# An attention and two MLP blocks on one core: when the first queries, the third weight unit and the last stores are issued

## The reference

```python
# block 1: attention. q, k, v: (4, 8, 1152, 64)
q_pool = q.reshape(B, H, S // 2, 2, D).mean(axis=3)         # 576 pooled queries
scores = matmul(q_pool, k.transpose(0, 1, 3, 2)) / sqrt(D)
attn = exp(scores - max(scores)); attn /= sum(attn) + 1e-9
x = matmul(attn, v)                                         # -> (4, 576, 512)

# block 2: gated MLP that mixes tokens
h = gelu(x @ w_in)                                          # 512 -> 1024
u, v = h[..., :512], h[..., 512:]
v_n = (v - mean) / sqrt(var + 1e-6) * g_ln
v_s = einsum('ts,bsd->btd', w_sg, v_n) + b_sg
x = x + (u * v_s) @ w_out

# block 3: token mixing, then channel mixing
u = x + (relu(x^T @ w_tok1) @ w_tok2)^T                     # 576 -> 256 -> 576
out = u + relu(u @ w_ch1) @ w_ch2                           # 512 -> 1536 -> 512
```

## Time and profile before

| | |
|---|---|
| three runs | 991.78, 992.71, 993.19 us |
| the profiled execution, its own time | 991.15 us |
| its span in the trace | 989.3 us |
| PE busy | 976.6 us, 99% of the span |
| DVE, ACT, POOL busy | 565.7, 462.1, 378.8 us |
| granted TensorE clock | 0.999 of full |
| DMA engines, mean share | 85% in the first fortieth, 30 to 50% through attention, near 0 after |

### The profile page before, as it was taken

The page is one execution under the profiler, slowest core; times in us unless marked ns, Lnnn a source line. Parts: engine busy times, 40 slices in busy tenths (PEclk is TensorE's granted clock), DMA queues, the critical chain, the costliest instruction groups (busy, mean ns, idle before and its releaser), DMA issues.

```text
span 989.3 us, 22718 instructions
## 1 busy us (share of the span) xinstructions
PE 976.6 (99%) x8810; PEld 806.3 (81%) x8810; DVE 565.7 (57%) x1166; ACT 462.1 (47%) x878; POOL 378.8 (38%) x295
## 2 busy tenths in 40 slices
PE   7999999999999999999999999999999999999998
PEld 6777777777777776689999999888888888888898
DVE  5787888888888877787575847545113122131121
ACT  5788888888888877844332423312111111011110
POOL 5777777777777786440000004484000000000000
PEclk9999999999999999999999999999999999999999
DMA  8544444444444433310000002141001001010010
GB/s 251 145 121 120 119 119 119 116 117 111 116 118 117 119 83 97 116 40 1 1 1 1 1 1 57 37 146 43 1 1 43 1 0 42 0 40 3 0 44 22
DMA packets 34459, 65.00 MB, mean 66 GB/s; under 512 B 6256, under 2 KB 15344, under 8 KB 34416
## 3 DMA queue, kind: packets, MB, share of 16 engines
q1 hardware_dynamic: 33968, 63.82, 22.9%
q10 hardware_dynamic: 448, 0.56, 0.2%
HBM read 42.93 MB, written 4.72 MB: 48 GB/s over the span
## 4 chain that ended last, share of the span: by engine, by line
PE 93%; DVE 3%; issue 1%; DMA 1%; POOL 1%; ACT 1%; SPq 0%; ACTq 0%; DVEq 0%; POOLq 0%
PE ps L894 18%; PE ps L895 18%; PE ps L896 18%; PE ps L835 15%; PE ps L823 11%; PE ps L740 8%; PE ps L811 1%; DVE prob L1406 1%; PE ps L813 1%; PE ps L812 1%; DMA k_plain<-in_k 1%; PE ps L950 1%; PE ps L788 1%; POOL prob L627 1%; PE ps L900 0%
## 5 line engine op out<-in xcount | busy, mean ns | idle before, releaser
L627 POOL TENSOR_SCALAR prob<-prob,rsum 128x1152 f32<-128x1152 f32 x144 | 177.7, 1234 | 94.1 <-DVE rsum L1415 94.0
L1406 DVE TENSOR_SCALAR_CACHE_REDUCE prob<-ps 128x1152 f32<-128x1152 f32 x128 | 173.8, 1358 | 65.8 <-PE ps L823 57.6
L1180 ACT ACTIVATE prob<-prob,nmax 128x1152 f32<-128x1152 f32 x144 | 181.3, 1259 | 9.7 <-DVE nmax L1389 4.4
L835 PE MATMUL ps<-pT,v_sb 128*64 128x288 f32 x1152 | 170.6, 418 | 0.0
L1653 DVE SCALAR_TENSOR_TENSOR f_l<-ps,f_h 128x512 fp32r<-128x512 f32 (+1 forms) x60 | 38.3, 638 | 222.4 <-ACT f_h L1350 222.4
L1350 ACT ACTIVATE f_h<-ps 128x512 fp32r<-128x512 f32 (+1 forms) x60 | 33.3, 555 | 254.7 <-PE ps L896 254.7
L1173 ACT ACTIVATE pT<-ps 128x512 f32<-128x512 f32 (+1 forms) x288 | 111.9, 436 | 64.6 <-PE ps L740 56.0
L823 PE MATMUL ps<-k_over,q_over 64*128 64x288 f32 x720 | 127.1, 309 | 0.0
L823 PEld LDWEIGHTS ps<-k_over,q_over 64*128 64x128 f32 x720 | 98.7, 184 | 26.3 <-DVE prob L1406 25.8
L740 PE MATMUL ps<-ident,prob 64*128 64x64 f32 x2592 | 105.2, 222 | 4.1 <-POOL prob L627 2.7
L740 PEld LDWEIGHTS ps<-ident,prob 64*128 64x128 f32 x2592 | 100.7, 139 | 8.9 <-issue 8.9
(11 more groups left out here) (158 smaller groups left out, 2150.6 us busy)
## 6 DMA issues: line engine op xcount, KB each, us to landing
q_raw<-in_q SPq DMA_DIRECT2D x15, 640.0 KB, 5.0
v_sb<-in_v SPq DMA_DIRECT2D x32, 288.0 KB, 2.9
k_raw<-in_k SPq DMA_DIRECT2D x15, 576.0 KB, 4.0
k_over<-kh SPq DMA_DIRECT2D x30, 144.0 KB, 2.5
k_over<-kl SPq DMA_DIRECT2D x30, 144.0 KB, 2.6
out_x<-xT SPq DMA_DIRECT2D x4, 1024.0 KB, 4.2
q_over<-qh SPq DMA_DIRECT2D x30, 128.0 KB, 2.3
q_over<-ql SPq DMA_DIRECT2D x30, 128.0 KB, 2.4
```

Source lines behind the costliest of these rows:

```text
L627: g.tensor_scalar(sl, sl, rsum[:, s:s + 1], 0.0, ALU.mult, ALU.add).then_inc(norm_done, 1)
L835: ins = te.matmul(ps[PH * c:PH * c + PH, ACC_BANK, 0:n], v_sb[:, a, j, :], pT[:, a, j, c * n:c * n + n], start=(j == 0), stop=(j == KB - 1))
L1180: sc.activation(sl, sl, ACT.Exp, scale=-1.0, bias=nmax[:, s:s + 1], accum_out=esum[:, s:s + 1]).then_inc(exp_done, 1)
L1406: ve.tensor_scalar(prob[:, PROB_BUF[s], :].rearrange("p (c n) -> p c n", c=SCORE_BANKS), ps[:, b0:b0 + SCORE_BANKS, 0:CK], -SCALE, BIG, AL ...
```

## The change

1. The queries of tiles 0 and 1 of the first pair are loaded apart: tile 0's ahead of the keys, tile 1's behind them, with a semaphore of their own (`q_next_in`). DVE adds tile 0's halves, POOL tile 1's, and PE's step 1 waits for `q_next_summed`.
2. Head B's keys for `k_plain` are issued ahead of head B's queries. POOL's sum of head B's queries moves from before the first `norm` to behind it. `q_two_b` gets a place of its own beside the rest, since it is now read later.
3. Weight unit 2 is loaded one pair earlier, and units 0 and 1 are split in steps 6 and 7 instead of 7 and 8.
4. Of the last four stores ACT issues the second and the fourth.

```diff
         def load_a(eng, rows, k_to):
-            eng.dma_start(q_two[rows, :, 0:2 * P], q[0, 0:PH, :, 0:2 * P]).then_inc(q_two_in, 16)
+            eng.dma_start(q_two[rows, :, 0:P], q[0, 0:PH, :, 0:P]).then_inc(q_two_in, 16)
             for m in range(2):
                 cols = slice(m * 2 * CK, (m + 1) * 2 * CK)
                 eng.dma_start(k_to[rows, cols], k[0, 0:PH, cols]).then_inc(k_a_in[m], 16)
+            eng.dma_start(q_two[rows, :, P:2 * P], q[0, 0:PH, :, P:2 * P]).then_inc(q_next_in, 16)
             eng.dma_start(q_two[rows, :, 2 * P:4 * P], q[0, 0:PH, :, 2 * P:4 * P]).then_inc(q_rest_in, 16)
+
+        def store_left(eng, e):
+            eng.wait_ge(y_free, Y_N + KT_N * B + e + 1)
+            eng.dma_start(out_v[:, e:NP:KT_N, CN:SQ], xT[:, e:NP:KT_N, CN:SQ]).then_inc(stored, 16)
@@ SyncE
             sp.dma_start(q_tail[:, :, :], q[0, :, :, 4 * P:QC]).then_inc(q_tail_in, 16)
+            sp.dma_start(k_plain[up, :], k[0, PH:P, :]).then_inc(k_b_in[0], 16)
             for rows in (up, low):
                 sp.dma_start(q_two_b[rows], q[0, PH:P, :, 0:4 * P]).then_inc(q_two_b_in, 16)
-            sp.dma_start(k_plain[up, :], k[0, PH:P, :]).then_inc(k_b_in[0], 16)
@@
             body(NP - 3, 1)
+            load_w(2)
             body(NP - 2, 0, more=False)
-            for u in range(2, U_WO):
+            for u in range(3, U_WO):
                 load_w(u)
@@
-            for e in range(KT_N):
-                sp.wait_ge(y_free, Y_N + KT_N * B + e + 1)
-                sp.dma_start(out_v[:, e:NP:KT_N, CN:SQ], xT[:, e:NP:KT_N, CN:SQ]).then_inc(stored, 16)
+            for e in range(0, KT_N, 2):
+                store_left(sp, e)
@@ GpSimd, in body()
+                    if first and s == 2:
+                        pool.wait_ge(q_two_b_in, 32)
+                        g.tensor_tensor(q_two_b_sum, q_two_b[:, 0, :], q_two_b[:, 1, :], ALU.add).then_inc(q_two_b_summed, 1)
@@
+            second = slice(P, 2 * P)
+            pool.wait_ge(q_next_in, 32)
+            g.tensor_tensor(q_two_sum[:, second], q_two[:, 0, second], q_two[:, 1, second], ALU.add).then_inc(q_next_summed, 1)
@@
-            pool.wait_ge(q_two_b_in, 32)
-            g.tensor_tensor(q_two_b_sum, q_two_b[:, 0, :], q_two_b[:, 1, :], ALU.add).then_inc(q_two_b_summed, 1)
@@
-            body(NP - 3, 1, w0=0, w=(7, 8))
-            body(NP - 2, 0, w0=1, w=(7, 8))
+            body(NP - 3, 1, w0=0, w=(6, 7))
+            body(NP - 2, 0, w0=1, w=(6, 7))
@@ TensorE, in first_scores()
+                if s == 1:
+                    pe.wait_ge(q_next_summed, 1)
@@ ScalarE, at its end
+            for e in range(1, KT_N, 2):
+                store_left(act, e)
@@ VectorE
-            early = slice(0, 2 * P)
+            early = slice(0, P)
```

More of the change, by code:

```diff
@@ L142, in build @@
         q_two = sb(ctx0, "q_two", [P, 2, 4 * P])
+        q_two_sum = sb(ctx0, "q_two_sum", [P, 4 * P])
+        sb(ctx0, "beside_q_two_b", [P, KB * SQ - 12 * P])
         q_two_b = sb(ctx0, "q_two_b", [P, 2, 4 * P])
-        q_two_sum = sb(ctx0, "q_two_sum", [P, 4 * P])
         ctx0.close()
@@ L227, in build @@
         k_a_in = [sem(f"k_a_in{m}") for m in range(2)]
+        q_next_in = sem("q_next_in")
         q_rest_in = sem("q_rest_in")
+        q_next_summed = sem("q_next_summed")
         q_two_in = sem("q_two_in")
```

## The result

| | before | after |
|---|---|---|
| runs, median | 992.93 us (991.78 to 993.75, 5 runs) | 987.72 us (987.32 to 988.29, 5 runs) |
| the profiled execution, its own time | 991.15 us | 987.32 us |
| its span, granted clock | 989.3 us, 0.999 | 985.5 us, 1.0 |

The ratio is 0.9946, interval 0.9935 to 0.9958: 5.2 us less, where 3.65 were forecast. One thing is odd in this table and carries the whole case: the two profiled executions are 3.83 us apart, the two medians 5.2. The median of the kernel after is 0.4 us above its profiled execution, that of the kernel before 1.8 us above its own.

The account below looks back on a forecast made before the run. PE was taken to bound the kernel (93% of the chain that ended last), so only its waits counted: -3.15 - 0.5 + 0 = -3.65 us, 992.71 to 989.06, forecast 989.1 us; own range 988.4 to 989.9, 8 in 10 988.0 to 990.6.

Parts of the forecast that it names:

- Part 3: Weight units, last three pairs: PE's two stalls on POOL's `norm` go, 0.74 and 2.41 us; term -3.15 us, bounds -3.15 to -2.2.
- the last margin: Last pair, tile 1: POOL's `norm` done at 390.3, PE wants it at 391.3, so 1.0 us to spare.
- that rival: Last pairs: POOL's slips beyond three 1.0 us margins only move the stall; half the gain gone, 991.0 us; chance 8%.
- Parts 1 and 2: First pair, queries by tile and head B's keys earlier: less waiting, term -0.5 us, bounds +0.4 to -0.9.
- the start of the tail scores: First pair, PE's step 4: start at about 11.95 instead of 12.55, without the 0.89 us wait for head B's keys.
- the slower rival: First pair: head B's queries, issued behind the keys, arrive too late for POOL; 993.0 us or more; chance 2%.
- Part 4: Last stores, issued by two engines: DMA engines already 98% busy, term 0, between -0.4 and +0.3 us.
- The step that failed: From profile to runs: the -3.65 us, being stretches of waiting, taken alike from profiled 991.15 and median 992.71 us.
- the second stall: Last pair: POOL's `norm` late because unit 2's load was issued late; PE idle 2.18 us, loss 2.41 us.
- more than forecast: Start and end of the kernel: both reach their best bounds, -3.15 - 0.9 - 0.4, giving 988.3 us; chance 6%.
- -3.15 at best (steady pace everywhere): Weight units, last three pairs: the best bound of their term, reached if every pair takes the undisturbed 24.97 us.
- the rival has 14: First pair wins nothing since step 1's queries come late: -3.15 + 0.2, 989.8 us; chance 14%.

Follow-up runs that it names:

- e2_units: Kernel before with only the third weight unit loaded one pair earlier and units 0 and 1 split in steps 6 and 7: 987.97 us, ratio 0.9955.
- e8_after: The changed kernel once more, without any edit, beside runs of the kernel before: 988.44 us, ratio 0.9956.
- e9_fill28: Kernel before plus 28 small identity transposes where PE stands still in the last pair; the wait for the load stays: 991.16 us, ratio 0.9986.
- e10: The changed kernel with DVE's wait for `g_col` moved from ahead of the gated MLP to its first mix: 987.33 us, ratio 0.9951.
- e11: Kernel before with only the weight-unit change, plus DVE's wait for `g_col` moved to the gated MLP's first mix: 987.8 us, ratio 0.9954.
- e3_start: Kernel before with only the first pair's changes: queries loaded by tile, head B's keys ahead of its queries, their sum behind the first `norm`: 992.85 us, ratio 1.0000.
- e12_units_keys_defer: Kernel before with head B's keys first, the weight-unit change and DVE's deferred `g_col` wait: 987.68 us, ratio 0.9953; one of six runs took 4411.8 us.
- e1_base: Plain copy of the kernel before, no edit, timed beside it: 992.75 us, ratio 1.0008.
- e7_steps: Kernel before with only the splits of weight units 0 and 1 moved to steps 6 and 7; third unit still loaded late: 992.02 us, ratio 0.9994.
- e4_stores: Kernel before with only ACT issuing the second and fourth of the last stores: 992.89 us, ratio 1.0001.

## Why the prediction was wrong, by its steps

**Part 3: the trace's arithmetic was right.** Forecast -3.15, measured between the two profiles -3.19. The low part of unit 0 started at 350.00 (said: 350.1), and the last margin is 1.0 us as worked out; the stall was not moved, which settles that rival. The three periods take 74.87 us again in e2_units (74.88) and e8_after (74.86). The profiled execution as a whole was forecast at 987.5 and took 987.32.

**Parts 1 and 2: the mechanism is seen, the size is not shown.** Forecast -0.5, measured -0.55 between the two profiles, and the start of the tail scores was met within 0.03 us; but there is luck in this. The term rests on the 0.89 us that PE waited for head B's keys, and that was the longest such wait of nine profiles with the old start: 0.27 to 0.77 us in six of them, and none in e2_units and e9_fill28. The 24 turns of the warm-up, which come first, took 4.12 to 5.35 us from profile to profile. So the place of pair 13 lies at 326.57 to 327.30 with the old start (median 327.03) and at 326.51 to 327.14 with the new one (four profiles, middle 326.6; the changed kernel alone has 326.55 and 327.14): 0.4 us, inside the scatter. The runs give 0.5 or 0.3 with part 4 (e10 against e11) and none in e3_start. The earliest place of all, 326.03, is that of e12_units_keys_defer, without part 1: one profile, which hints that part 1 costs something. Unforeseen was that one DMA issue more delays the keys of the next pair and puts 0.53 us of waiting behind ACT; it is contained in the -0.55. Head B's queries (the slower rival) never bound: POOL took them at 13.56 without a wait.

**Part 4: right.** 3.16 and 3.13 us after the last sum, where 3.11 stood before: 0. The DMA engines are 98% busy at 216 GB/s with one issuer and at 215 with two.

**The step that failed is the carry-over to the runs.** It read: "Since all terms are stretches of waiting, they are the same in both". They are not. The profiled execution of before (991.15 us, clock 0.999) is of the kind of the 26 in 69 in which the clock held; the median lies among the 43 in which PE's standstill brought the 1.2 GHz level. For them the second stall costs not 2.41 us but some 1.8 more. The kernel after has no standstill there and its clock held in all 11 of its runs. So the missing term is -1.4 us for the medians: (992.93 - 991.15) - (987.72 - 987.32) = 1.78 - 0.40. With it -3.65 becomes -5.0, and -5.2 was measured. This sum closes by its making, since it uses the medians that it explains. What doesn't: the 26 undisturbed runs of before have a median of 991.3, and 3.65 less is 987.7, where 987.72 was measured; the clock's price, 1.8 us between the two groups, is borne out by 1.5 and 2.57 in two traces and 1.4 in e9_fill28. No rival of the prediction had this mechanism: "more than forecast" came nearest in time, 988.3, by bounds that were not reached.

The sign that was there: the profile was 1.56 us faster than the median of the three runs, more than any term but one. I told that difference and let it stand as an offset of both kernels. With "why is the median slower than the trace" asked of each long stall, the range would have reached to -5. The bound "-3.15 at best (steady pace everywhere)" was the same error: it bounds the profiled execution, not the runs. (A slip without weight: the sum of the chances took 13 where the rival has 14.)

What stays open: why the clock falls in some executions and holds in others after nearly the same standstill. e1_base stood 2.45 us and kept it, e7_steps stood 2.1 and lost it. The size of the whole gain is known no better than to a microsecond: 5.2 us in the first comparison, 4.4 by the ratio in its repeat, e8_after.

## What to carry to other kernels

Compare the profiled execution with the runs' median before working anything out: where they are a microsecond or more apart, the trace may be of a lucky execution (here before) or an unlucky one (here e4_stores), and a term of the sum may be missing from it. The mean clock of each run tells which. In this kernel, whose TensorE is full, a standstill of 2 to 3 us cost its own length plus what the clock cost behind it (1.8 us in 6 of 10 executions), so it was worth more to remove than its row said; in another, look for the same. Where the wait can't be removed, small matmuls of the identity put into it, sized from a measured row, may keep the clock: 28 of them made this kernel 1.4 us faster, 60 gave nothing. And a term at the start of a program should be read from several profiles, since one of them can hold the longest wait of nine.

## What the runs showed of the hardware

- After a standstill of 2.14 us (e7_steps) and 3.03 us (e4_stores) in otherwise full work the granted clock fell to 0.50 (1.2 GHz), for some 3.5 and 7 us; after 2.18, 2.25 and 2.45 us (before, e3_start, e1_base) it held. By their mean clock it fell in 43 of 69 executions of the kernel before. With the standstill filled it held in 24 of 24.
- A 2 KB load took 3.0 to 3.2 us in six profiles and 3.3 or 3.4 in five, and that decided over 0.9 us of the stretch behind it.
- The same 24 transposes of 128x128 at the program's start took 4.12 to 5.35 us in fourteen profiles, with a granted clock of 1.00 shown in all.
- In a row of small transposes of 64x64, each further one takes (3.82 - 1.92) / (58 - 28) us = 63 ns.
- Last stores issued by one engine or two: 216 and 215 GB/s, DMA engines 98% busy both times, no gain.
